# Gram masks of a recurrence on VectorE instead of GpSimd, VectorE's slots laid out anew, and large loads in pieces of 2 KB

## What is computed

```python
def _attn_ref(r, k, v, w, a, b):
    state = zeros((B, H, D, D))
    for t in range(S):
        y[:, :, t] = einsum('bhd,bhde->bhe', rt, state)
        Sa = einsum('bhde,bhe->bhd', state, at)
        state = state * wt[:, :, None, :] - einsum('bhd,bhe->bhde', Sa, bt) + einsum('bhd,bhe->bhde', vt, kt)

# x = y as (3072, 320)
# experts: top 2 of 8 by noisy logits; out[rows of e] += weight * (relu(x @ w1[e]) @ w2[e])
# last part: h = x @ w_in; out = max(0.01 * h, h) @ w_out
```

## Time and profile before

| | us |
|---|---|
| median of 3 runs | 1638.34 |
| the runs | 1636.05 to 1650.76 |
| the profiled execution | 1636.78 |
| its span | 1635.0 |

### The profile page before, as it was taken

The page is one execution under the profiler, slowest core; times in us unless marked ns, Lnnn a source line. Parts: engine busy times, 40 slices in busy tenths (PEclk is TensorE's granted clock), DMA queues, the critical chain, the costliest instruction groups (busy, mean ns, idle before and its releaser), DMA issues. The chain is left out here.

```text
span 1635.0 us, 40604 instructions
## 1 busy us (share of the span) xinstructions
PE 1341.4 (82%) x16814; PEld 1217.7 (74%) x16814; DVE 909.5 (56%) x1553; ACT 655.1 (40%) x1451; POOL 304.8 (19%) x253
## 2 busy tenths in 40 slices
PE   3549698888979796004999999999993999999998
PEld 3437586666868585004999999999993889889887
DVE  4857557492663401504777777778772453554533
ACT  3314334343434122203666666666661333333332
POOL 3316132241411110570000000000003210110000
PEclk9957767686687665556999999999997999999999
DMA  6753554748352222735676676676661110110000
GB/s 153 176 112 100 126 157 119 202 119 193 113 145 81 76 71 64 266 120 172 216 259 216 218 255 218 219 253 218 222 214 53 53 32 17 49 38 10 16 17 16
DMA packets 149248, 219.58 MB, mean 134 GB/s; under 512 B 61210, under 2 KB 120474, under 8 KB 145722
## 3 DMA queue, kind: packets, MB, share of 16 engines
q1 hardware_dynamic: 132143, 163.84, 34.4%
q10 hardware_dynamic: 9891, 27.97, 5.8%
q0 software_dynamic: 7088, 25.89, 4.8%
HBM read 185.49 MB, written 42.34 MB: 139 GB/s over the span
## 5 line engine op out<-in xcount | busy, mean ns | idle before, releaser
L1232 DVE TENSOR_TENSOR gf<-psM,low 128x512 f32<-128x512 f32 x96 | 66.4, 692 | 179.3 <-ACT low L1270 179.3
L331 DVE TENSOR_TENSOR prod<-Tl,Lt 128x1 f32<-128x1 f32 (+30 forms) x186 | 142.9, 768 | 38.0 <-DMA Lt<-lscr 31.9
L1075 PE MATMUL psE<-w2h,hh 128*128 128x320 f32 x496 | 155.9, 314 | 0.0
L1270 ACT ACTIVATE low<-psM 128x512 f32<-128x512 f32 x96 | 57.5, 599 | 242.6 <-PE psM L1328 242.6
L1077 PE MATMUL psE<-w2h,hl 128*128 128x320 f32 x496 | 153.5, 309 | 0.0
L1076 PE MATMUL psE<-w2l,hh 128*128 128x320 f32 x496 | 153.4, 309 | 0.0
L1060 PE MATMUL psE<-xh,w1h 128*128 128x256 f32 x496 | 141.6, 285 | 5.6 <-DVE w1l L965 5.6
L1061 PE MATMUL psE<-xl,w1h 128*128 128x256 f32 x496 | 141.5, 285 | 0.0
L1062 PE MATMUL psE<-xh,w1l 128*128 128x256 f32 x496 | 141.5, 285 | 0.0
L965 DVE TENSOR_TENSOR w2l<-w2t,w2h 128x320 fp32r<-128x320 f32 x248 | 122.1, 492 | 10.8 <-ACT w2h L960 10.8
L1307 PE MATMUL psM<-woh,gh 128*128 128x320 f32 x384 | 120.1, 313 | 2.9 <-DVE gl L965 2.5
(11 more groups left out here) (170 smaller groups left out, 3378.9 us busy)
## 6 DMA issues: line engine op xcount, KB each, us to landing
w2t<-in_w_dram SPq DMA_DIRECT2D x31, 1280.0 KB, 6.2
w1t<-in_w_dram SPq DMA_DIRECT2D x31, 1024.0 KB, 8.1
w1t<-in_w_dram SPq DMA_DIRECT2D x62, 256.0 KB, 8.8
Vd<-in_vG_dram ACTq DMA_DIRECT2D x22, 640.0 KB, 6.2
xs<-xsort SPq DMA_DIRECT2D x31, 320.0 KB, 5.7
ysort<-ys POOLq DMA_DIRECT2D x31, 320.0 KB, 4.3
xsort<-in_zer_dram SPq DMA_DIRECT2D x15, 640.0 KB, 8.3
RV<-in_rvE_dram ACTq DMA_DIRECT2D x22, 416.0 KB
```

The source lines that it names most:

```text
L331: mark(nc.vector.tensor_tensor(prod[:, 0:t, 0:t], Tl[:, 0:t, CH - t:CH], Lt[:, t:t + 1, CH - t:CH].to_broadcast([128, t, t]), ALU.mult))
L1075: mm(o, hh[:, f, sl], w2h[:, f, :], start=(f == 0), stop=False)
```

## The change

1. The masks of `GvT`, `Gpb` and of `LkT` for blocks 1 to 5 go from GpSimd to VectorE, with semaphores `v_gv`, `v_gp`, `v_lk` instead of `g_gv`, `g_gp`, `g_lk`. The four masks of `LkT` of block 0 stay on GpSimd.
2. VectorE's order in a round is a new one: `y_out(k - 2)`, the mask on `Gpb` of round k - 1, then by slot as in the diff. The suffix is first in slot 0, the decay last in slot 3.
3. GpSimd makes B in slot 0, and K and then A in slot 1 (it was A and B in slot 1, K in slot 2).
4. P, U, A, B, K, `RV` and `Vd` are laid out in HBM with the pieces outermost: a row of P, U, A, B or K comes in four pieces of 2048 or 2064 bytes, one of `RV` in two of 2048, one of `Vd` in two of 2560.

```diff
+        def by_run(ap):
+            return ap.rearrange("r p x -> p r x")
...
-                sp.dma_start(P[:, :, :], wR[s]).then_inc(q["l_p"], 16)
+                sp.dma_start(P[:, :, :].rearrange("p (r g) t -> p r (g t)", r=4), by_run(wR[s])).then_inc(q["l_p"], 16)
...
-                sp.dma_start(AT[:, s % 3, :, :, :], aE[s]).then_inc(q[f"l_a{s % 3}"], 16)
+                sp.dma_start(AT[:, s % 3, :, :, :].rearrange("p r g t -> p r (g t)"), by_run(aE[s])).then_inc(q[f"l_a{s % 3}"], 16)
...
             for k in range(NK):
                 s, c = slot(k)
-                mask_gv(k)
-                if c < 2 and s + 1 < NS_:
-                    mask_lk(s + 1, 2 * c)
-                    mask_lk(s + 1, 2 * c + 1)
+                if c == 0 and s + 2 < NS_:
+                    make_B(s + 2, 0)
+                    make_B(s + 2, 1)
                 if c == 1 and s + 2 < NS_:
-                    for j in range(2):
-                        make_A(s + 2, j)
-                        make_B(s + 2, j)
-                if c == 2 and s + 2 < NS_:
                     make_K(s + 2)
-                mask_gp(k)
+                    make_A(s + 2, 0)
+                    make_A(s + 2, 1)
...
+            def mask_gp(k):
+                dve.wait_ge(q["a_Gp"], k + 1)
+                t = Gpb[:, :, :, :].rearrange("p b h m -> p (b h) m")
+                nc.vector.tensor_tensor(t, t, tiled(neg_m[:, :], 128), ALU.mult).then_inc(q["v_gp"], 1)
...
-            steps = {0: 14, 1: 12, 2: 18, 3: 64}
+            dve.wait_ge(q["l_c"], 80)
             for k in range(NK + 2):
                 s, c = slot(k)
...
                 if k < NK and c == 0:
                     T = inverse(s + 1) if s + 1 < NS_ else iter(())
-                    if k:
-                        decay(s - 1)
                 if k >= 2:
                     y_out(k - 2)
+                if 1 <= k <= NK:
+                    mask_gp(k - 1)
                 if k >= NK:
                     continue
-                for i in range(steps[c]):
-                    if c == 0 and i == 8 and s + 2 < NS_:
+                if c == 0:
+                    if s + 2 < NS_:
                         suffix(s + 2)
-                    if c == 1 and i == 11 and s + 2 < NS_:
+                    invert(10)
+                    mask_gv(k)
+                    if s + 1 < NS_:
+                        mask_lk(s + 1, 0)
+                    invert(17)
+                    if s + 1 < NS_:
+                        mask_lk(s + 1, 1)
+                elif c == 1:
+                    invert(10)
+                    mask_gv(k)
+                    if s + 1 < NS_:
+                        mask_lk(s + 1, 2)
+                    if s + 2 < NS_:
                         prefix(s + 2)
-                    next(T, None)
+                    invert(8)
+                    if s + 1 < NS_:
+                        mask_lk(s + 1, 3)
+                elif c == 2:
+                    invert(6)
+                    mask_gv(k)
+                    invert(6)
+                else:
+                    invert(6)
+                    mask_gv(k)
+                    if s + 1 < NS_:
+                        decay(s)
...
+    for n in ("aE", "bE", "kE", "wE", "wR"):
+        a[n] = a[n].reshape(NS_, EP, 4, -1).transpose(0, 2, 1, 3)
```

More of the change, by code:

```diff
@@ L243, in make_K, with mask_lk @@
                 i.then_inc(q["e_K"], 1)
-            def mask_lk(s, c):
-                pool.wait_ge(q["a_G"], round_lk(s, c) + 1)
-                t = LkT[:, s % 2, c, :, :, :].rearrange("p h g t -> p (h g) t")
+            def mask_lk(c):
+                pool.wait_ge(q["a_G"], round_lk(0, c) + 1)
+                t = LkT[:, 0, c, :, :, :].rearrange("p h g t -> p (h g) t")
                 tt(t, t, pos_m[:, :].rearrange("p (o t) -> p o t", o=1).to_broadcast([128, 8, CH]), ALU.mult).then_inc(q["g_lk"], 1)
[L250 to L258, removed]
             make_A(0, 0)
@@ L264, in _ @@
             for c in range(4):
-                mask_lk(0, c)
+                mask_lk(c)
             for j in range(2):
@@ L378, in _, with invert @@
                 pass
-            steps = {0: 14, 1: 12, 2: 18, 3: 64}
+            dve.wait_ge(q["l_c"], 80)
             for k in range(NK + 2):
                 s, c = slot(k)
+                def invert(n):
+                    for _ in range(n):
+                        next(T, None)
                 if k < NK and c == 0:
                     T = inverse(s + 1) if s + 1 < NS_ else iter(())
-                    if k:
-                        decay(s - 1)
                 if k >= 2:
                     y_out(k - 2)
+                if 1 <= k <= NK:
+                    mask_gp(k - 1)
                 if k >= NK:
                     continue
-                for i in range(steps[c]):
-                    if c == 0 and i == 8 and s + 2 < NS_:
+                if c == 0:
+                    if s + 2 < NS_:
                         suffix(s + 2)
-                    if c == 1 and i == 11 and s + 2 < NS_:
-                        prefix(s + 2)
-                    next(T, None)
+                    invert(10)
[11 more added lines that the diff above has]
+                    if s + 2 < NS_:
+                        prefix(s + 2)
+                    invert(8)
[10 more added lines that the diff above has]
+                        decay(s)
         @block.scalar
@@ L726, in _ @@
                     read_S(k - 1, 0)
-                    pe.wait_ge(q["g_gp"], k)
+                    pe.wait_ge(q["v_gp"], k)
                     add_B(k - 1)
@@ L748, in _ @@
                     read_S(k - 1, 1)
-                    pe.wait_ge(q["g_gv"], k)
+                    pe.wait_ge(q["v_gv"], k)
                     pe.wait_ge(q["o_y"], 4 * k - 1)
@@ L1415, in layouts @@
     a["cst"] = c
+    for n in ("aE", "bE", "kE", "wE", "wR"):
+        a[n] = a[n].reshape(NS_, EP, 4, -1).transpose(0, 2, 1, 3)
+    a["rvE"] = a["rvE"].reshape(NK, EP, 2, -1).transpose(0, 2, 1, 3)
+    a["vG"] = a["vG"].reshape(NK, 128, 2, -1).transpose(0, 2, 1, 3)
     for n, m in (("noise", "moe_noise"), ("w1", "moe_w1"), ("w2", "moe_w2"), ("w_in", "moe2_w_in"), ("w_out", "moe2_w_out")):
```

42 lines of the change are left out of this document (26 added, 16 removed).

## The result

The changed kernel took 1659.72 us (median of 4 runs, 1652.79 to 1666.45) beside 1641.57 us of the kernel before: a ratio of 1.0119, with a 95% interval of 1.0075 to 1.0164. The profiled execution took 1661.25 us (span 1659.5), where that of before took 1636.78. Forecast were 1652 us and a range of 1620 to 1672. Slower by over 1% had 0.40, within 1% had 0.45.

What follows compares the result with a forecast made beforehand. TensorE was taken to set the pace of the recurrence, its idle 83 us being what VectorE's order could win or lose. Terms -2.7 + 7.1 + 3.6 + 36.9 - 22.7 - 3.0 - 3.9 gave +15.3, so 1652.1 us; range 1620 to 1672.

Steps and rivals of the forecast that it cites:

- The five waits go: -22.7 us: Block ends: with the decay moved into slot 3, TensorE's five waits for S0T vanish, -22.7 us.
- y_out behind suffix and inverse: Blocks 1 to 3, slot 0: P's landing to y_out 14.9 us unhindered, 19.9 with GpSimd, was 7.3; +36.9 us in all.
- SP's chain ahead of P: SP's queue at block starts: the DMAs before P's issue hardly move relative to the round, +0.55 us a block.
- The pieces: Large loads: 2 KB pieces bring them in faster, -0.9 us a load and -2.7 us at the start.
- Rival (d): Large loads: the pieces bring nothing, at the start or in four blocks; 1658 us, chance 0.12.
- GpSimd: Slot 0: make_B and make_K hold up VectorE's small inverse products, 5 us a block.
- Rival (a): Slot 0: GpSimd holds up nothing, since B and K land late; 1629 us, chance 0.17.
- I let slot 1 go on as before: Slot 1 after the transposes: U meets an empty queue, and the slot was taken to run unchanged.
- I let the wait for the inverse go: Before the last block: with the inverse out early, TensorE's wait for TT goes, -3.0 us.
- The clock need not fall at the boundary: -3.9: Start of block 4: 10 us of TensorE work at 0.61 would take about 6.1 us at full clock, -3.9 us.
- Rival (c): Slot 1: the long stall costs TensorE its full clock, +5.4 us a block; 1668 us, chance 0.16.
- Rival (b): Slot 1: TensorE holds 2.4 GHz, shrinking its 25 us by some 8 us; 1605 us, chance 0.10.

Runs made afterwards that it cites:

- Experiment 3: The kernel before with only the decay moved into slot 3, after 12 half-steps of the inverse: 1644.54 us, ratio 1.0013.
- experiment 9: The kernel before with the decay moved into slot 3 and P's load issued ahead of from_lanes, to_lanes and to_blocks: 1649.87 us, ratio 1.0037.
- experiment 4: The changed kernel with slot 0's 27 half-steps of the inverse and two small masks ahead of the suffix: 1639.94 us, ratio 0.9986 to the kernel before.
- Experiment 7: The changed kernel with ScalarE's RV and Vd loads of slot 3 issued half a round later: 1651.99 us, ratio 1.005 to the kernel before.
- experiments 1 and 2: The kernel before with only the 2 KB pieces: 1643.55 us, ratio 1.002; the changed kernel with whole rows instead of pieces: 1664.1 us, ratio 1.0133.
- experiment 5: The changed kernel with all masks back on GpSimd, in GpSimd's order of the kernel before: 1660.5 us, ratio 1.0125 to the kernel before.
- experiment 6: The changed kernel with P's load issued ahead of from_lanes, to_lanes and to_blocks in SP's queue: 1642.87 us, ratio 1.0 to the kernel before.
- experiments 9 and 12: 12: the new chain with slot 3's RV and Vd loads issued half a round later, 1638.19 us, ratio 0.9972; 9: see experiment 9.
- the new chain: The changed kernel with the inverse ahead of the suffix, SP issuing P first and to_lanes last: 1626.11 us, ratio 0.9903 to the kernel before.

## Why the forecast came out as it did

The time lay in the range and 7.7 us above the value. In the profiled executions the forecast difference was +15.3 us, the measured one +24.5. By blocks, from the starts of TensorE's first rounds (before 179.6, 275.4, 367.1, 466.1, 548.7; after 189.0, 293.2, 391.2, 489.5, 578.7 us; ends 642.3 and 668.0):

| stretch | forecast us | measured us |
|---|---|---|
| start and block 0, less one decay | +3.5 | +9.4 |
| blocks 1 to 3: 36.9, less three decays | +23.3 | +14.0 |
| block 4: decay, clock | -8.4 | +6.6 |
| block 5: TT | -3.0 | -4.3 |
| sum | +15.4 | +25.7 |

A decay is counted here as a fifth of 22.7 us; the five waits were 5.5, 4.6, 5.6, 5.4 and 1.7 us. The sum of the profiled executions is 9 us short, the most in block 4.

**The decay.** "The five waits go: -22.7 us" held as far as the waits go, and failed as a gain. Experiment 3 shows that they covered other work: taken away alone, they are worth nothing (1.0013). In experiment 9, 14.8 of the 22.7 us came back as waits for TT and xT, and TensorE was busy 16.4 us longer. I had priced a stall at its length; it was worth what the next late thing left of it.

**y_out behind suffix and inverse.** The mechanism was right, and it is the change's main cost (experiment 4: 20 us). Forecast were transposes at R'+40.5, 12.3 us later in each of three blocks, 36.9 in all; measured were 43.4, 38.7 and 38.3, so 15.1, 10.7 and 10.1, 35.9 in all. That 36.9 came so close is luck, since its terms were wrong and cancelled:

- *SP's chain ahead of P.* Forecast +0.55 us a block, P at R'+13; measured P at R'+16.4, 16.5 and 16.6. L158 began at R'-1.8, even before the R'+0.2 of the forecast; the chain took 18.2 us instead of 12.8. I had moved the chain in time and not asked what it would run beside. Experiment 7 shows that it was the RV and Vd loads.
- *The pieces.* Forecast -0.9 us a load (its own figures give 3.5 us instead of 4.5, so -1.0) and -2.7 at the start; measured nothing (experiments 1 and 2, AT awaited for 17.1 us again). I had read 293 against 226 from a window of 3 us in which other, smaller loads ran as well; in this kernel the window from 12 to 24 us, all in pieces, moved 183 GB/s at 0.87. The Trainium skill, page "DMA: Bandwidth & Descriptors", section "Specifications", asks for at least 512 bytes for line rate. The runs agree: both sizes are above that, and 2 KB against 8 KB made no difference. Rival (d) named it, with 0.12.
- *GpSimd.* Forecast 5 us a block of held-up products; block 1 had them (2.04, 1.85 us and smaller ones; P's landing to the transposes took 20.0 us, forecast 19.9), blocks 2 and 3 had none, since B was there only when y_out had begun (14.6 us in both, against the 14.9 of the unhindered sum). Rival (a) was right there. The prediction had said that it is wrong if y_out comes within 15 us of P; in these two blocks it did.

Two more readings follow. The waits for xT were to be three of 12 to 20 us; they are 6.5, 8.4 and 12.1 us, since TensorE itself came to slot 1 later (the first slots of these blocks took 30.6, 24.2 and 23.2 us, where they took 19.6, 19.6 and 22.8). And "I let slot 1 go on as before" was wrong in the other direction: from the transposes to the end of the slot it took 24.8, 24.4 and 24.2 us instead of 27.5, 25.5 and 29.9, which is most of why the blocks lost 14.0 us and not 23.3.

**Block 0.** Gpb cost 8.5 us (forecast 7.1) and y_out 3.8 (forecast 3.6). The start gave none of its 2.7.

**TT.** I let the wait for the inverse go (-3.0). It went before the last block and came in blocks 1 to 4, 16.0 us in all, for the same reason that P was late: `to_blocks` stands behind the stretched `to_lanes`. Block 4 has 6.4 us of it.

**The clock.** "The clock need not fall at the boundary: -3.9" was said of block 4 and gave nothing: its first slot had a mean clock of 0.81 instead of 0.76, but TensorE was busy 18.8 us in it as against 18.7, and the slot was 7.5 us longer, 6.4 of them for TT. Its last slot was busy 16.9 us at 0.65 instead of 15.2 at 0.77, which took back the 1.7 us of its decay. The forecast had no term for the clock of the other blocks; the first slot of block 1 ran at 0.67 instead of 0.76, of block 2 at 0.71 instead of 0.76, busy 22.4 and 21.0 us instead of 18.7 each. Rival (c), a loss of clock after the long stall of slot 1, didn't happen: slot 1 of blocks 1 to 3 ran at 0.59, 0.60 and 0.55 before and at 0.59 in each after. Rival (b) didn't happen either.

**The masks.** Counted at nothing, and experiment 5 agrees within its interval.

## What to carry to other kernels

A wait on the bounding engine is worth only what remains of it when the next late thing is moved up too: take it away alone on the chip before it goes into a sum. When a chain of small DMAs shifts by a few microseconds, list the large loads it will then run beside. Where an engine waits for a load, put the independent work ahead of the wait and not behind it; here that alone was worth 1.3%, and with P issued first and the transfers that nothing hangs on issued last, some 2% (0.9903 against 1.0119).

## What the runs showed of the hardware

- The four DMAs of `to_lanes` (small pieces out of HBM) took 3.5 us on SP's queue in block 1 with RV and Vd moved away (experiment 7; 2.7 and 2.3 in blocks 2 and 3), 6.7 us beside the 1056 KB of RV and Vd (7.3 and 7.7), and 13.2 us beside these and P (experiment 6; 13.1 and 10.9).
- A load of 0.86 MB by 104 rows of 8 KB is as fast as one by 416 pieces of 2 KB: from issue to VectorE's next instruction 8.5, 6.8 and 7.6 us against 7.8, 7.6 and 7.3.
- A VectorE product of 64 elements with two inputs in SBUF took 0.23 us alone (block 1) and 2.11 us when it began beside a GpSimd product (block 0). By the Trainium skill, page "SBUF — State Buffer", section "SBUF: two separate sides", one of the two then fully blocks. The rows agree: in block 1 the product of 81 elements begins at 222.84, behind GpSimd's at 222.59, and ends at 224.88, when the first of GpSimd's two (4.33 us together) is over.
- The same 10812 matmuls were busy for 454 us in one profiled execution and 475 in another, at mean granted clocks of 0.72 and 0.70. That is as much as the waits that these experiments removed. Part of it is spread between executions. In experiments 9 and 12, whose medians of 12 runs say the same, it is the most likely reason why less idle time brought no time; no experiment changed the clock alone.
- Some of TensorE's idle time looks like a wait for its own code. The DMA view has a queue of the kind "instruction", with 85 packets of 16 KB in the recurrence of the kernel before. TensorE's 5.57 us wait at 205.08, whose releaser is "issue", holds one of them, in a stretch in which the other queues are busy (before, TensorE's timeline, then the DMA queue in 199.5 to 205.1 us):

```profile
205.08 0.89 PE L532 MATMUL psA<-S0T,AT 40*32 40x40 f32 x58 [5.57 <-issue]
...
q8 instruction: 1, 0.02, 1.5%
```

The packet starts near 202.4, and TensorE goes on 1.4 us after it has landed. In the fourteen traces TensorE has 144 waits of over 1.2 us with the releaser "issue" between 100 and 660 us; in 128 of them such a packet lands, at most 2 us ahead of their end. All rows of "issue" from 100 us on add up to 29.2 us before, 36.3 us in experiment 3, and 43.7 of the 68.8 us of idle time that the new chain has left. That the code comes late where loads are dense is a reading of these rows; no experiment tests it.
